# Partial sums of a seven-product matmul seeded from PSUM bank to bank, with the last product deferred

## What is computed

```python
def _moe_ref(x, w_gate, w1, w2):
    N, D = x.shape                  # 1536, 512
    E = w_gate.shape[1]             # 8 experts, hidden width 1024
    ...                             # P: gates, normalised 8 times over rows and columns
    for e in range(E):
        h = np.maximum(x @ w1[e], 0.0)
        ye = h @ w2[e]
        out += P[:, e:e + 1] * ye
```

## Time and profile before

| what | value |
|---|---|
| median of three runs | 1344.09 us |
| the three runs | 1341.1, 1344.09, 1344.49 us |
| span of the profiled execution, first to last instruction | 1339.7 us |
| PE busy | 1312.7 us, 98% |
| DVE busy | 840.0 us, 63% |
| ACT busy | 569.0 us, 42% |
| POOL busy | 290.4 us, 22% |
| DMA over the span | 109.84 MB, mean 82 GB/s |
| chain of waits, by engine | PE 88%, DVE 5%, ACT 3% |

### The profile page before, as it was taken

One profiled execution on the slowest core, in us unless ns is written; L12 is line 12 of the kernel. 1 busy time (PEld: TensorE's weight loads), 2 busy tenths in 40 slices (PEclk: granted clock), 3 DMA queues, 4 the chain that ended last, 5 costly groups with the idle time before them and its releaser, 6 DMA issues.

```text
span 1339.7 us, 24715 instructions
## 1 busy us (share of the span) xinstructions
PE 1312.7 (98%) x9435; PEld 760.1 (57%) x9435; DVE 840.0 (63%) x1486; ACT 569.0 (42%) x871; POOL 290.4 (22%) x249
## 2 busy tenths in 40 slices
PE   6999999999999999999999999999999999999997
PEld 3776667665455456445545644554564465556675
DVE  5999999786576347436634742662474275567994
ACT  6999999742143114304311430431242043225762
POOL 4667666613002000300200030030003000121111
PEclk8999999999999999999999999999999999999999
DMA  9444441051011011001101100110110023368960
GB/s 240 95 118 108 107 116 47 26 206 63 1 63 64 1 63 63 0 1 65 59 0 63 63 0 5 71 50 0 63 63 0 13 74 110 131 209 295 320 225 21
DMA packets 51920, 109.84 MB, mean 82 GB/s; under 512 B 5504, under 2 KB 9128, under 8 KB 51856
## 3 DMA queue, kind: packets, MB, share of 16 engines
q1 hardware_dynamic: 49392, 105.58, 24.9%
q0 software_dynamic: 2240, 3.35, 0.7%
q10 hardware_dynamic: 224, 0.02, 0.0%
HBM read 93.57 MB, written 17.34 MB: 83 GB/s over the span
## 4 chain that ended last, share of the span: by engine, by line
PE 88%; DVE 5%; ACT 3%; issue 2%; DMA 1%; SPq 0%; POOL 0%; ACTq 0%; POOLq 0%; DVEq 0%
PE ps L1689 14%; PE ps L1693 14%; PE ps L1692 14%; PE ps L1715 11%; PE ps L1718 11%; PE ps L1717 11%; PE ps L1614 4%; PE ps L1602 2%; PE ps L1604 2%; PE ps L1586 1%; ACT probsT_hi L826 1%; PE ps L1624 1%; PE ps L1626 1%; PE ps L1628 1%; ACT A L814 1%
## 5 line engine op out<-in xcount | busy, mean ns | idle before, releaser
L1715 PE MATMUL ps<-x_hi,w_hi 128*128 128x384 f16 x896 | 292.1, 326 | 0.1
L1718 PE MATMUL ps<-x_hi,w_lo 128*128 128x384 f16 x896 | 292.1, 326 | 0.0
L1717 PE MATMUL ps<-x_lo,w_hi 128*128 128x384 f16 x896 | 292.1, 326 | 0.0
L1693 PE MATMUL ps<-w_hi,h 128*128 128x512 f16 x768 | 291.0, 379 | 0.0
L1692 PE MATMUL ps<-w_lo,h 128*128 128x512 f16 x768 | 291.0, 379 | 0.0
L1689 PE MATMUL ps<-w_hi,h 128*128 128x512 f16 x768 | 291.0, 379 | 0.0
L1328 DVE SCALAR_TENSOR_TENSOR x<-ps,gate_now,x 128x512 f32<-128x512 f32 x84 | 63.1, 751 | 251.6 <-PE ps L1693 250.7
L945 ACT ACTIVATE x1s<-ps 128x384 f32<-128x384 f32 x64 | 30.4, 475 | 326.2 <-PE ps L1718 326.2
L637 POOL TENSOR_TENSOR wf<-wf 128x1024 f32<-128x1024 f32 x8 | 18.8, 2355 | 633.0 <-PE ps L1718 622.4
L962 ACT ACTIVATE h<-parts 128x1152 f16<-128x1152 f32 x64 | 74.4, 1163 | 136.1 <-DVE parts L1284 136.1
L1693 PEld LDWEIGHTS ps<-w_hi,h 128*128 128x128 f16 x768 | 75.1, 98 | 90.7
(11 more groups left out here) (228 smaller groups left out, 2232.3 us busy)
## 6 DMA issues: line engine op xcount, KB each, us to landing
wf<-w1a SPq DMA_DIRECT2D x32, 512.0 KB, 6.0
w_stage_in<-w2a SPq DMA_DIRECT2D x8, 2048.0 KB, 8.8
w_in<-w1b SPq DMA_DIRECT2D x4, 2048.0 KB, 8.9
w_in<-w2b SPq DMA_DIRECT2D x4, 2048.0 KB, 9.9
w_in_b<-w1b SPq DMA_DIRECT2D x4, 2048.0 KB, 11.2
w_in_b<-w2b SPq DMA_DIRECT2D x4, 2048.0 KB, 10.4
rows<-blank SPq DMA_DIRECT2D x1, 6682.0 KB, 21.1
qk_in<-kT SPq DMA_DIRECT2D x32, 192.0 KB, 4.3
```

The costliest lines, as they stand in the source:

```text
L1693: last = pe.matmul(acc, a_lo, b_hi, start=False, stop=(m == n - 1))
L1715: pe.matmul(group_bank(g, role), w_hi, x_hi, start=(opens and kt == 0), stop=False, skip_group_check=not opens)
L1717: pe.matmul(group_bank(g, role), w_hi, x_lo, start=False, stop=False, skip_group_check=not opens)
L1718: last = pe.matmul(group_bank(g, role), w_lo, x_hi, start=False, stop=(kt == 1), skip_group_check=not opens)
```

## The change

The products are made in another order, two copies go from one PSUM bank to another, and the product P3 of each group is made in the next group.

- Role 0 holds P1, then P1 + P2 = C11, as before.
- Role 1 holds P7, then P7 + P4. P7 alone is copied to SBUF first (`parts[..1]`, `p7_kept`).
- Role 2 is filled by ACT with a copy of P1 out of role 0 (`b_seeded`), and the matmuls of P6 add onto it: U2 = P1 + P6. ACT copies U2 to SBUF (`parts[..0]`, `u2_kept`), and P5 is added in the bank.
- Role 3 is filled by ACT with a copy of role 2 (`c_seeded`, after P5), and P3 of the group is added onto it in the next group, behind that group's P1 and P7. In the last group of an expert no next group follows: `last_product(NGROUPS - 1)` stands right behind P5, ahead of the second stage.
- DVE has two sums left (C21 and C22). C12 is read directly out of PSUM: its `h_hi` (`take_c12`) and `h_lo` (`split_c12`) are separate operations of 384 columns, and those of C21 and C22 have 768 columns instead of 1152. Both halves of ACT's and DVE's work on C12, C21 and C22 now stand in the next group.
- In expert 0, PE first makes three matmuls of 128 columns into the bank of role 3, behind a wait for the last softmax (`probs_ready`). The block sums of `x` on POOL, and their casts on ACT and DVE, come in the order 5, 1, 3, 2 instead of 1, 2, 3, 5.
- Waits for "all products of the expert done" name P3's semaphore. `parts` has two thirds of its size and `x1s` is gone.

The diff, cut to its core:

```diff
-X_SUMS, X_BLOCKS = (1, 2, 3, 5), (0, 4, 6)
-X_SUM_AT = {2: 1, 1: 2, 3: 3, 5: 4}
+X_SUMS, X_BLOCKS = (5, 1, 3, 2), (0, 4, 6)
+X_SUM_AT = {5: 1, 2: 2, 1: 3, 3: 4}
...
@@ ACT, expert @@
+                def take_c12(g):
+                    act.wait_ge(p3_done, e * NGROUPS + g + 1)
+                    act.activation(h[:, b, 0, i, 1, :], group_bank(g, 3), ACT.Relu).then_inc(hi12_ready, 1)
+                def take_last_two(g):
+                    act.wait_ge(c22_ready, e * NGROUPS + g + 1)
+                    act.wait_ge(c21_ready, e * NGROUPS + g + 1)
+                    act.activation(h[:, b, 0, i, 2:4, :], parts[g % 2][:, :, :], ACT.Relu).then_inc(hi2_ready, 1)
...
-                    act.wait_ge(mm1_done, products_done + 1)
-                    reached(act, u3_ready, groups_done)
-                    act.activation(x1s[:, :], group_bank(g, 0), ACT.Copy).then_inc(p1_copied, 1)
+                    act.wait_ge(p1_done, groups_done + 1)
+                    if g > 0:
+                        act.wait_ge(lo11_ready, groups_done)
+                    act.activation(group_bank(g, 2), group_bank(g, 0), ACT.Copy).then_inc(b_seeded, 1)
+                    act.wait_ge(p7_done, groups_done + 1)
+                    reached(act, lo2_ready, groups_done - 1)
+                    act.activation(parts[g % 2][:, 1, :], group_bank(g, 1), ACT.Copy).then_inc(p7_kept, 1)
                     between(0)
-                    act.wait_ge(mm1_done, products_done + 3)
-                    reached(act, lo3_ready, groups_done - 1)
-                    act.activation(parts[g % 2][:, 2, :], group_bank(g, 2), ACT.Copy).then_inc(p5_copied, 1)
+                    if g > 0:
+                        take_c12(g - 1)
+                        take_last_two(g - 1)
+                    act.wait_ge(p6_done, groups_done + 1)
+                    act.activation(parts[g % 2][:, 0, :], group_bank(g, 2), ACT.Copy).then_inc(u2_kept, 1)
                     between(1)
...
-                    act.wait_ge(c22_ready, groups_done + 1)
-                    act.wait_ge(c21_ready, groups_done + 1)
-                    act.wait_ge(c12_ready, groups_done + 1)
-                    act.activation(h[:, b, 0, i, 1:4, :], parts[g % 2][:, :, :], ACT.Relu).then_inc(hi3_ready, 1)
+                    act.wait_ge(p5_done, groups_done + 1)
+                    if g > 0:
+                        act.wait_ge(c21_ready, groups_done)
+                    act.activation(group_bank(g, 3), group_bank(g, 2), ACT.Copy).then_inc(c_seeded, 1)
+                take_c12(NGROUPS - 1)
+                take_last_two(NGROUPS - 1)
...
@@ DVE, expert @@
+                    if g > 0:
+                        split_c12(g - 1, groups_done - 1)
+                        split_last_two(g - 1, groups_done - 1)
...
+                    dve.wait_ge(p4_done, groups_done + 1)
+                    dve.wait_ge(u2_kept, groups_done + 1)
+                    dve.tensor_tensor(now[:, 0, :], group_bank(g, 1), now[:, 0, :], ALU.add).then_inc(c21_ready, 1)
+                    dve.wait_ge(p7_kept, groups_done + 1)
+                    dve.wait_ge(c_seeded, groups_done + 1)
+                    dve.tensor_tensor(now[:, 1, :], group_bank(g, 2), now[:, 1, :], ALU.add).then_inc(c22_ready, 1)
...
@@ PE, expert @@
+                if first:
+                    pe.wait_ge(probs_ready, NTILES)
+                    for k in range(HT // P):
+                        pe.matmul(group_bank(0, 3)[:, k * P:(k + 1) * P], ones16[:, :], ones16[:, :],
+                                  start=(k == 0), stop=(k == HT // P - 1), skip_group_check=True)
+                def last_product(g):
+                    pe.wait_ge(c_seeded, e * NGROUPS + g + 1)
+                    x_parts(g, 6)
+                    group_product(g, 3, 6, 6, False, p3_done)
...
+                    if g >= 2:
+                        pe.wait_ge(c22_ready, groups_done - 1)
+                    group_product(g, 0, 0, 0, True, p1_done)
...
+                    if g >= 2:
+                        pe.wait_ge(lo12_ready, groups_done - 1)
+                    group_product(g, 1, 5, 5, True, p7_done)
+                    if g > 0:
+                        last_product(g - 1)
+                    pe.wait_ge(b_seeded, groups_done + 1)
+                    group_product(g, 2, 4, 1, False, p6_done)
...
+                    group_product(g, 0, 1, 4, False, p2_done)
...
+                    pe.wait_ge(p7_kept, groups_done + 1)
+                    group_product(g, 1, 2, 3, False, p4_done)
+                    pe.wait_ge(u2_kept, groups_done + 1)
+                    group_product(g, 2, 3, 2, False, p5_done)
...
+                last_product(NGROUPS - 1)
```

More of the change, by code:

```diff
@@ L265, in build @@
         tail_parts.close()
-        parts = [sb(f"parts{r}", [P, 3, HT], fp32) for r in range(2)]
+        parts = [sb(f"parts{r}", [P, 2, HT], fp32) for r in range(2)]
+        sb("after_parts", [P, 3, HT], fp32)
         w1_stage, w2_stage = (w1_in, w1_in_b), (w2_in, w2_in_b)
@@ L746, in _ @@
             with pool.Fori(2, E) as e:
-                pool.wait_ge(mm1_done, NM1 * e)
+                pool.wait_ge(p3_done, NGROUPS * e)
                 sum_w1(e)
@@ L1263, in expert @@
                     b, i = divmod(g, FH)
[L1264 to L1269, removed]
+                    groups_done = e * NGROUPS + g
+                    now = parts[g % 2]
                     if g > 0:
-                        split_rest(g - 1, groups_done - 1, before)
+                        split_c12(g - 1, groups_done - 1)
+                        split_last_two(g - 1, groups_done - 1)
                     dve.wait_ge(hi11_ready, groups_done + 1)
@@ L1362, in expert, with split_c12, split_last_two @@
                     find_slots(GROUPS - 1)
-            def split_rest(g, groups_done, now):
+            def split_c12(g, groups_done):
                 b, i = divmod(g, FH)
[L1367 to L1370, removed]
+                dve.wait_ge(hi12_ready, groups_done + 1)
+                dve.scalar_tensor_tensor(out=h[:, b, 1, i, 1, :], in0=group_bank(g, 3), scalar=0.0,
+                                         in1=h[:, b, 0, i, 1, :], op0=ALU.max, op1=ALU.subtract
+                                         ).then_inc(lo12_ready, 1)
+            def split_last_two(g, groups_done):
+                b, i = divmod(g, FH)
+                dve.wait_ge(hi2_ready, groups_done + 1)
+                dve.scalar_tensor_tensor(out=h[:, b, 1, i, 2:4, :], in0=parts[g % 2][:, :, :], scalar=0.0,
+                                         in1=h[:, b, 0, i, 2:4, :], op0=ALU.max, op1=ALU.subtract
+                                         ).then_inc(lo2_ready, 1)
             def turned_lo(t):
@@ L1705, in logit_columns, with group_product @@
                 return last
-            def group_product(g, role, a, k, opens):
+            def group_product(g, role, a, k, opens, done):
                 b, i = divmod(g, FH)
@@ L1719, in group_product @@
                                      skip_group_check=not opens)
-                last.then_inc(mm1_done, 1)
+                last.then_inc(done, 1)
             def expert(e, first, last_one):
                 pe.wait_ge(w1_lo_ready, NP * e + NP)
+                if first:
[3 more added lines that the diff above has]
+                                  start=(k == 0), stop=(k == HT // P - 1), skip_group_check=True)
@@ new lines, in x_parts @@
+                def x_parts(g, k):
+                    b, i = divmod(g, FH)
+                    if first and i == 0:
+                        pe.wait_ge(*((x7_lo_dve, len(X_SUMS) * b + X_SUMS.index(k) + 1) if k in X_SUMS else
+                                     (x7_lo_pool, len(X_BLOCKS) * b + X_BLOCKS.index(k) + 1)))
+                def last_product(g):
+                    pe.wait_ge(c_seeded, e * NGROUPS + g + 1)
+                    x_parts(g, 6)
+                    group_product(g, 3, 6, 6, False, p3_done)
@@ L1724, in expert @@
                 for g in range(NGROUPS):
-                    b, i = divmod(g, FH)
                     groups_done = e * NGROUPS + g
[L1728 to L1736, removed]
-                            freed = (lo11_ready, u3_ready, c12_ready, c21_ready)[n % 4]
-                            pe.wait_ge(freed, e * NGROUPS + n // 4 + 1)
@@ L1812, in expert @@
                         pe.wait_ge(columns_in, t)
-                        pe.matmul(ps[:, 3, 0:E], ones[:, :], column_sum[:, :], start=True, stop=True
+                        pe.matmul(ps[:, 0, 0:E], ones[:, :], column_sum[:, :], start=True, stop=True
                                   ).then_inc(columns_done, 1)
```

86 lines of the change are left out of this document (33 added, 53 removed).

## The result

The changed kernel takes 1350.28 us (median of four runs, 1347.89 to 1351.52) against 1344.24 us before. The ratio is 1.0049, with a 95% interval of 1.0033 to 1.0066: slower by 6.0 us, where +6.7 had been forecast. The profiled execution is the run of 1347.89 us and has a span of 1346.1 us, 6.4 us above that of before.

A forecast was written before the change was run, and what follows sets the result against it. PE, without idle time in the dense part, was taken as the bound. Stalls 6.1, small matmuls 0.2 and transposes 0.4 summed to +6.7 us: 1344.1 + 6.7 = 1350.8 us, 0.5% slower, range 1347.0 to 1356.0.

The forecast's parts named there:

- PE has nothing to give back in the dense part: Both stages of all experts: idle time before 384-column matmuls 0.1 us and less over 880 us, so relieving DVE gains nothing.
- Rival 1: Matmuls regain 2.5 ns each through less DVE work, 6.7 us in all, cancelling the stalls: 1344.1 us; chance 6%.
- The eight bare waits: Last group of each expert: P3 waits for the copy behind P5, stall 0.76 us, eight times: +6.1 us.
- The copy within PSUM: ACT's 384-column copy from bank to bank, taken as 0.49 us from the nearest rows.
- Rival 2: The copy from bank to bank is slow, 0.98 us, and group 0 stalls too: +13.4, 1357.5 us; chance 9%.
- the lower bound of 0.36: Shortest bank-to-bank copy on ACT, from the 96-column operation: 0.36 us, giving stalls of 0.63 us (+5.0).
- The transposes in expert 0: Transposes of `x`, one product earlier: PE there at 251.76, waits for DVE's `normalise_last` until 252.17: +0.4 us.
- The three small matmuls: Expert 0: three 128-column matmuls at a third of 0.1625 us each: +0.2 us.
- Seven groups out of eight cost nothing: Every group but each expert's last: next group's P1 and P7 hide the new waits; least margin 0.14 us.
- Rival 3: Each expert's stall slows the clock, 8 x 1.7 = 13.6 us more: 1364.4 us; chance 4%.
- The 4.4 us put on top of the span: Median of the runs lay 4.4 us above the profiled span before; the same was added to the forecast span.
- The lower end of the range: 1344.1 + 5.6 - 1.9 = 1347.8 us, lowered to 1347.0 for a part of the even cases.

The follow-up runs named there:

- The move by six matmuls: Changed kernel with each expert's last P3 put behind the second stage's first six matmuls: 1342.64 us, ratio 0.9996 to the kernel before.
- the enlarged copy: Changed kernel with a second ACT copy to spare SBUF columns ahead of each copy into role 3, in all 64 groups: ratio 1.0081 to the kernel before.
- the control: The changed kernel run once more with nothing altered: ratio 1.0050 to the kernel before, span 1350.5 us.

## Why the prediction was right

- **PE has nothing to give back in the dense part.** Right, and shown from two sides. Where DVE lost work, the pace of the matmuls stayed; where DVE got more than it ever had, it stayed too; and where all waits were taken out, the time came back to 0.9999 of before, and the dense part to within 0.17 us of it, which another place explains. Rival 1 has fallen. By the rule named with it in the Trainium skill ("TensorE: Matmul & The Clock Gate", "Wait — 56ns, not 53.3ns?"), the 2.5 ns are fixed for each matmul; the traces here agree, with 0.1625 us a step under DVE loads between 29 and 42 us in a first stage.
- **The eight bare waits.** Predicted at 0.37 + 0.49 + 0.06 = 0.92 us from start to start, measured at 0.89: 0.36 to the start of the copy, 0.47 for it, 0.06 to the matmul. The sum of +6.1 was +5.8. The move by six matmuls took the cost away and the enlarged copy added to it, so the wait is shown as the cause.
- **The copy within PSUM.** Taken at 0.49 us from the nearest rows, measured at 0.474. Rival 2 has fallen, and the lower bound of 0.36 too. The prediction held that the side of the write alone tells the copies apart, and took the longer of two SBUF rows. The Trainium skill ("ScalarE: Activation LUTs", "Step-by-step: what each stage is for") lets a write to PSUM be faster than one to SBUF; the traces agree, by 15 to 16 ns of 491 where ACT was idle before. That is 0.1 us in eight waits.
- **The transposes in expert 0.** +0.4 predicted, and the net is +0.4, but in two parts of which the prediction had one. DVE's release came when it said (5.10 us after P1's first start, 5.11 predicted). PE was ready 0.16 us earlier than it said, since the last head's small matmuls put it 0.63 us behind the products and not 0.80: a pause behind them that the kernel before has is gone. So the wait is 0.56 and not 0.41, and 0.17 is won in front of it. That they cancel is luck. The three small matmuls: 0.2 predicted, 0.17 measured.
- **Seven groups out of eight cost nothing.** Right for groups 1 to 6, wrong in one place. The step "In group 0 ACT first casts a quarter of w2 ... usable at 8.51, still 0.26 us early" counted seven products in group 0. It has six: its own P3 is deferred, and none of an earlier group stands in. P3 is due at 8 x 0.975 = 7.80, not at 8.775. With the prediction's own durations the copy is 0.7 us late in expert 1, where the transfer lands last. Measured: 0.19 us in the first profile, whose cast started 6.5 us after P1, and 0.60 in the control, with 6.9 us:

```profile
381.99 1.06 ACT L903 ACTIVATE w_hi<-w_stage_in 128x1024 f16<-128x1024 f32 x1 [2.32 <-DMA w_stage_in<-w2a]
382.95 0.47 ACT L981 ACTIVATE ps<-ps 128x384 f32<-128x384 f32 x1
```

  The slip was small because only one expert of seven has so late a transfer. In the others of the first profile the copy is usable 6.8 to 7.2 us after P1.
- **The clock.** Rival 3 has fallen. The eight stalls of 0.73 us left it at 1.00, those of 1.25 us with the enlarged copy too, and so did the inner stalls of that size in the kernel without the deferral, one in every 7.6 us, as in this stretch of expert 2 with seven of them:

```profile
513.21:566.17 52.96, 48.99 (x294) 28.20 (x295) 25.57 (x39) 26.57 (x52) 0.00 (x0) 1.00 0.11 40
```

  The Trainium skill ("TensorE: Matmul & The Clock Gate", "A second HAM failure mode: psum-queue depth-cycling") tells of a clock that oscillates with waits between groups; these runs don't show it at this size of gap.
- **The total.** +6.7 predicted, +6.4 in the spans, +6.0 in the medians. The one wrong step (+0.19) and the slightly shorter wait (-0.2) nearly cancel, which is luck as well. That the spans come so near is in part chance, since the control's lies 4.4 us higher. The 4.4 us put on top of the span for the median came out at 4.2, but the profiled execution itself took only 1.8 us more than its span; the rest is that it was the fastest of the four runs.
- **Two slips without weight.** 288 matmuls at the shorter form's pace are 46.8 us and not over 47 (the real pace of 512 columns, 0.216 us, makes 62). The lower end of the range takes off 1.9 us where the text gives 1.7.

## What to carry to other kernels

Where PE runs back to back, ask of every wait in its queue how much other work stands between the producer's last matmul and the consumer's first, and count that work in each place where the pattern begins or ends: a software pipeline is bare in its last turn and short of one step in its first. A round trip over ACT costs about 0.9 us here (0.36 + 0.47 + 0.06), so five or six matmuls of 384 columns cover it, and if independent ones exist (here those of the next stage) the cure is to reorder, not to make the copy faster. Relieving an engine that nobody waited for gained nothing here, and loading it again cost nothing in the matmuls' pace.

## What was not expected of the hardware

- The clock fell behind a single gap of 2.25 us. In the kernel without the deferral, PE stood idle for that long until 388.13 in expert 1 (2.58 us from start to start), and the clock was at 0.50 (1.2 GHz) from 389.5 to 392.9, 3.4 us with matmuls at 0.32 us each, shown below. After the gaps of 1.2 to 1.4 us in experts 2 to 7 it stayed at 1.00, and also after two gaps of 1.84 and 1.08 us in expert 0, 8 us apart (until 266.28 and 274.41). It is one fall in one execution:

```profile
389.50:392.90 3.40, 3.40 (x12) 1.53 (x11) 0.37 (x1) 0.52 (x2) 0.00 (x0) 0.50 0.00 0
```

- The low stretches at the kernel's start and in its tail are not the same from execution to execution. The first profile of the changed kernel has one of 3.4 us in the tail, the control one of 6.8 us. Near the start both have one of 6.8 us, but in the first profile the clock first reaches 1.00 at 8.9 us and the stretch begins at 12.4, in the control these are 14.6 and 28.3 us; with six matmuls ahead the clock reaches 1.00 at 17.6 us and no such stretch follows before the tail. Of the 4.4 us between two spans of the same program 3.1 arose before the dense part and 0.9 in the tail, where these stretches lie. That they are the whole cause isn't shown. The spread of 3.4 us in the runs of before is of the same size.
- The same program's transfer of `w2` in expert 1 was ready for the cast 6.5 us after P1 in one execution and 6.9 us in another, so a margin of a few tenths in front of a transfer's consumer isn't a margin.
- How long ACT takes for a copy depends on what stands in front of it. The same copy of 384 columns out of PSUM into SBUF took 491 to 492 ns where ACT had been idle and 473 ns where another operation stood right before it (8 and 56 times in the kernel before, line 945). A mean over both hides the 16 ns by which a write into PSUM was shorter.
